# A rational activation's reciprocal moved from ScalarE's logarithm and exponential to VectorE's reciprocal instruction

## The chip, the cores and the metric

One core of one Trainium2 chip runs the whole program. The metric is the device time of one execution in microseconds (us). VectorE is DVE in the profile, ScalarE is ACT, GpSimd is POOL, TensorE is PE.

## The reference

Three stages follow one another over 2 x 4096 = 8192 tokens of width 192: a causal seven-tap convolution along the sequence with softmaxed weights, a layer with a rational activation, and a layer with a squared ReLU. All data is float32.

```
out  = einsum('hk,bskhg->bshg', softmax(weight), windows of x)      # 7 taps
h    = out @ moe_w_in                                               # 192 -> 2048
P    = a[0] + a[1]*h + a[2]*h**2 + a[3]*h**3
Q    = 1.0 + abs(b[0])*abs(h) + abs(b[1])*h**2
g    = P / (Q + 1e-06)
x2   = g @ moe_w_out                                                # 2048 -> 192
y    = (s * relu(x2 @ moe2_w_in)**2 + b2) @ moe2_w_out              # 192 -> 2048 -> 192
```

The change concerns the division in g: 8192 x 2048 reciprocals, which is 128 instructions of 128 partitions x 1024 elements.

## The kernel before

The tokens are cut into 16 tiles of 512 (two batches by eight pieces of the sequence, taken in pairs), and the inner width of 2048 into 8 units of two blocks of 128. So there are 128 units for each layer. A unit n of layer 1 is a tile of 128 x 1024 values of h in PSUM, and every operation on it is one instruction of 128x1024. Everything stays in SBUF and PSUM; only x, the weights and the output are moved by DMA.

Each engine has its own hand-written program (`@block.tensor`, `@block.scalar`, `@block.vector`, `@block.gpsimd`, `@block.sync`), in which a function `phase` goes through the eight units j of a tile; `run` calls it for tiles 0 and 1 written out, for the 12 tiles in the middle in a hardware loop, and for four phases at the end (the last two tiles and two that only empty the pipeline). Semaphores order the engines; inside an engine the order is that of the text. At its step n the work is skewed:

- PE (step n): `first_product` of layer 1 for unit n into `h1` (ten 128x512 matmuls, L314 to L318), the second product of layer 2 for unit n-13 (sixteen matmuls of 192 columns, L340), the first product of layer 2 for unit n-12 (ten, the same lines), the second product of layer 1 for unit n-3 (ten, L327 to L331). `h1` is one buffer: PE waits before `first_product` of unit n until VectorE has finished L615 of unit n-1 (`t3_done`). Layer 2 starts 12 units behind layer 1.
- ScalarE (step n): `a3*h+a2` (L468), `|b1|*|h|` (L470), the rounded high part `gh` of unit n-2 (L477), then for unit n the absolute value of VectorE's product (L480), its logarithm with 1+eps added (L482), the exponential of the negated logarithm, a first estimate of 1/Q (L485), then for layer 2 ReLU (L489) and square (L492).
- VectorE (step n): `(|b1||h| + |b0|) * h` (L610), `t*h` (L612), `(t+a1)*h` (L615), then pieces of the convolution for the next pair of tiles where the table `TAPS_AT` puts them (L510, L513, L521, L524), then for unit n-1 two refining steps, `q = (Q+eps)*r` (L649) and `r = (2-q)*r` (L651), and `g = (P)*r` (L655). At tile bounds it also splits the layer's sums into high and low parts (L570 to L585) and forms the output (L622).
- GpSimd (step n): `gl = g - gh` of unit n-2 (L297).

The buffers `q_buf`, `r_buf` and `num_buf` have two slots each, `gh` and `gl` too. The estimate L485 writes the slot of `r_buf` that `gl` of two units earlier has read, so ScalarE waits on `gl_ready` ahead of it. `w_abs` holds both the result of L470 and the logarithm, so L470 waits on `r0_ready` of the unit before.

Of the kernel before, what the change touches and what calls it, by code (L numbers as in the profile page):

```python
# [8 lines left out]
HALO = TAPS - 1  # L9
EPS_SUM = 1e-9  # L10
EPS_Q = 1e-6
LN_EXP_TABLES = 6

ALU = mybir.AluOpType
ACT = mybir.ActivationFunctionType
# [5 lines left out]
def counted(count):  # L21

    return max(count, 0) if isinstance(count, int) else count


def conv_rational_relu2_kernel(nc, x_main, x_tail, weight, w_in1, w_out1, a, b, w_in2, w_out2, s, b2, out):
# [45 lines left out]
    with ExitStack() as ctx:  # L72
# [6 lines left out]
        def sem(name):  # L79
            return ctx.enter_context(nc.semaphore(name))  # L80
# [19 lines left out]
        w_abs = work1[:, 0]  # L100
        t_buf = work1[:, 7]
        num_buf = [work1[:, 1], work1[:, 2]]
        q_buf = [work1[:, 3], work1[:, 4]]
        r_buf = [work1[:, 5], work1[:, 6]]
# [35 lines left out]
        one_eps = coef[:, 8:9]  # L140
# [23 lines left out]

        h1_ready, t_ready, w_ready = sem("h1_ready"), sem("t_ready"), sem("w_ready")
        z_done, t2_done, t3_done, q_ready = sem("z_done"), sem("t2_done"), sem("t3_done"), sem("q_ready")
        ln_done, r0_ready = sem("ln_done"), sem("r0_ready")
        e_done, r1_done, g_ready = sem("e_done"), sem("r1_done"), sem("g_ready")
        gh_ready, gl_ready, out1_done = sem("gh_ready"), sem("gl_ready"), sem("out1_done")

        h2_ready, u_ready, g2_ready, out2_done = sem("h2_ready"), sem("u_ready"), sem("g2_ready"), sem("out2_done")
# [12 lines left out]
        def raw_tail(c):  # L184

            return raw_w1_tail_early[:, c] if c.stop <= 2 * TOK else raw_w1_tail_late[:, c.start - 2 * TOK:c.stop - 2 * TOK]

        def in_h2(n):

            return isinstance(n, int) and n < SKEW and n % 2 == 1  # L190


        def unit(n):
            return not isinstance(n, int) or 0 <= n < NU

        def tile(t):
            return not isinstance(t, int) or 0 <= t < TILES

        def first(t):
            return isinstance(t, int) and t == 0  # L200

        def second(t):
            return isinstance(t, int) and t == 1
# [5 lines left out]
        def run(eng, phase):  # L209


            for t in range(2):
                phase(t * UNITS, t, t // 2, t % 2)
            with eng.Fori(1, TPB - 1) as i:
                n0 = eng.snap(i * (2 * UNITS))
                t0 = eng.snap(i * 2)
                for parity in range(2):
                    phase(n0 + parity * UNITS, t0 + parity, i, parity)
            for t in range(TILES - 2, TILES + 2):
                phase(t * UNITS, t, t // 2, t % 2)  # L220
# [205 lines left out]
        @block.scalar  # L426
        def _(act):


            act.dma_start(cw[:, :, :], weight).then_inc(cw_loaded, 16)  # L430
            act.add_instruction(mybir.InstLoadActFuncSet(name=nc.get_next_instruction_name(),
                                                         engine=mybir.EngineType.Activation,
                                                         act_func_set_id=LN_EXP_TABLES, ins=[], outs=[]))

            def high_of_weight(dst, raw):
                nc.scalar.copy(dst, raw).then_inc(w_hi_ready, 1)

            def high_of_w1(piece):
                c = PIECES[piece]
                act.wait_ge(w1_loaded[piece], 16)  # L440
                high_of_weight(w1_hi[:, c], raw_w1[:, c])
                act.wait_ge(w1t_loaded[piece], 32)
                high_of_weight(w1_tail_hi[:, c], raw_tail(c))

            act.wait_ge(cw_step, 1)
            nc.scalar.activation(cw[:, :, :], cw[:, :, :], ACT.Exp).then_inc(cw_exp, 1)
            high_of_w1(0)
            act.wait_ge(coef_loaded, 64)
            nc.scalar.activation(coef[:, 4:6], coef[:, 4:6], ACT.Abs).then_inc(coef_ready, 1)
            act.wait_ge(v1_loaded, 16)  # L450
            high_of_weight(v1_hi[:, :, :], raw_v1[:, :, 0:P])
            high_of_weight(v1_tail[:, :, 0, :], raw_v1[:, :, P:D])
            act.wait_ge(coef_ready, 2)

            def phase(n0, t, i, parity):
                for j in range(UNITS):
                    n, m = n0 + j, n0 + (j - SKEW)
                    buf = j % 2
                    if j == X2_STEP and tile(t - 1):

                        act.wait_ge(out1_done, counted(t * UNITS))
                        act.wait_ge(x2_tail_lo_ready, counted(t - 1))
                        nc.scalar.copy(x2_sum, o1_tail[TAIL:P, :]).then_inc(x2_tmp_ready, 1)
                    h_flat = h2_flat if in_h2(n) else h1_flat
                    if unit(n):
                        act.wait_ge(h1_ready, counted(n + 1))
                        act.wait_ge(t3_done, counted(n))
                        nc.scalar.activation(t_buf, h_flat, ACT.Identity, bias=a2, scale=a3).then_inc(t_ready, 1)  # L468
                        act.wait_ge(r0_ready, counted(n))
                        nc.scalar.activation(w_abs, h_flat, ACT.Abs, scale=b1_abs).then_inc(w_ready, 1)  # L470
                    if first(t) and j == 0:
                        high_of_w1(1)
                        high_of_w1(2)
                    if unit(n - 2):
                        act.wait_ge(g_ready, counted(n - 1))
                        act.wait_ge(out1_done, counted(n - 3))
                        nc.scalar.copy(gh[:, buf, :], r_buf[buf]).then_inc(gh_ready, 1)  # L477
                    if unit(n):
                        act.wait_ge(z_done, counted(n + 1))
                        nc.scalar.activation(q_buf[buf], q_buf[buf], ACT.Abs).then_inc(q_ready, 1)  # L480
                        act.wait_ge(q_ready, counted(n + 1))
                        nc.scalar.activation(w_abs, q_buf[buf], ACT.Ln, bias=one_eps).then_inc(ln_done, 1)  # L482
                        act.wait_ge(ln_done, counted(n + 1))
                        act.wait_ge(gl_ready, counted(n - 1))
                        nc.scalar.activation(r_buf[buf], w_abs, ACT.Exp, scale=-1.0).then_inc(r0_ready, 1)  # L485
                    if unit(m):
                        act.wait_ge(h2_ready, counted(m + 1))
                        act.wait_ge(g2_ready, counted(m))
                        nc.scalar.activation(u_relu, h2_flat, ACT.Relu).then_inc(u_ready, 1)  # L489
                        act.wait_ge(u_ready, counted(m + 1))  # L490
                        act.wait_ge(out2_done, counted(m - 1))
                        nc.scalar.activation(g2[buf], u_relu, ACT.Square).then_inc(g2_ready, 1)  # L492
                    if first(t) and j == 4:
                        act.wait_ge(w2_loaded, 16)
                        high_of_weight(w2_hi[:, :], raw_w2)
                    if second(t) and j == 0:
                        act.wait_ge(w2t_loaded, 32)
                        high_of_weight(w2_tail_hi[:, :], raw_w2)

            run(act, phase)  # L500

        @block.vector
        def _(dve):
# [94 lines left out]
            def phase(n0, t, i, parity):  # L598
                for j in range(UNITS):
                    n = n0 + j  # L600
                    buf = j % 2
# [43 lines left out]

                    q, r, num = q_buf[1 - buf], r_buf[1 - buf], num_buf[1 - buf]
                    if unit(n - 1):
                        dve.wait_ge(r0_ready, counted(n))
                        nc.vector.scalar_tensor_tensor(q, q, one_eps, r, ALU.add, ALU.mult).then_inc(e_done, 1)  # L649
                        dve.wait_ge(e_done, counted(n))  # L650
                        nc.vector.scalar_tensor_tensor(r, q, 2.0, r, ALU.subtract, ALU.mult,  # L651
                                                       reverse0=True).then_inc(r1_done, 1)
                        dve.wait_ge(r1_done, counted(n))
                        dve.wait_ge(t3_done, counted(n))
                        nc.vector.scalar_tensor_tensor(r, num, a0, r, ALU.add, ALU.mult).then_inc(g_ready, 1)  # L655
                    if j == X2_STEP and tile(t - 1) and not second(t):
# [2 lines left out]
                    if first(t) and j == 5:  # L659
                        dve.wait_ge(colsum_ready, 1)  # L660
                        nc.vector.tensor_scalar(bias_row[:, :], o2[:, 0, 0, 0:D], b2_col, None,
                                                ALU.mult).then_inc(bias_row_ready, 1)

            run(dve, phase)


# [30 lines left out]
```

## Time and profile before

| | |
|---|---|
| median of 3 executions | 1336.07 us (1335.62 to 1336.43) |
| the profiled execution | 1336.83 us |
| its span, first to last instruction | 1335.0 us |
| PE busy | 1259.8 us (94%) |
| DVE busy | 1160.5 us (87%) |
| ACT busy | 1098.3 us (82%) |
| POOL busy | 333.9 us (25%) |
| mean granted TensorE clock | 0.982 of full speed |

Busy times are sums over one profiled execution. An engine's busy share is an average over the start, the loop and the end; the stretches are told apart in the rows below. Idle time is put down to the instruction that ended it, so a row of waits names who was late.

### The profile page before, as it was taken

To read this page: it belongs to the slowest core of one execution; us is meant where nothing else is said; L and a number is where in the kernel's file an instruction comes from. 1 tells how busy PE (TensorE), PEld (TensorE's weight loads), DVE (VectorE), ACT (ScalarE), POOL (GpSimd) and SP (SyncE) were. 2 spreads that over 40 slices of the span, in tenths; PEclk is the share of its full clock that TensorE was granted. 3 is DMA by queue.
4 is the path that set the end of the run, shared out by engine and by line. 5 is a ranking of instruction groups with operands and counts; after the bars stand their busy time and mean duration, and the time that the engine had idled before them with its cause. 6 is when DMAs were issued, how large, how long until landed. Compare 5 with 4: busy or idle time off the path is not lost.

```text
span 1335.0 us, 16225 instructions
## 1 busy us (share of the span) xinstructions
PE 1259.8 (94%) x5920; PEld 1069.3 (80%) x5920; DVE 1160.5 (87%) x1073; ACT 1098.3 (82%) x1053; POOL 333.9 (25%) x145
## 2 busy tenths in 40 slices
PE   3665899999999999999999999999999999999998
PEld 2544688888888888888888888888888888888887
DVE  7999999998899989999899989999899998978810
ACT  4766788888888888888888888888898888888833
POOL 4233222222222222222222222222222222222200
PEclk9787899999999999999999999999999999999999
DMA  5310100001000100001000010001000000000000
GB/s 134 103 32 0 24 1 12 1 1 36 0 12 0 36 0 0 12 0 36 0 12 0 0 36 0 12 0 36 0 0 12 0 12 1 13 1 13 0 13 12
DMA packets 17885, 20.40 MB, mean 15 GB/s; under 512 B 1472, under 2 KB 13760, under 8 KB 17600
## 3 DMA queue, kind: packets, MB, share of 16 engines
q1 hardware_dynamic: 17712, 20.00, 5.5%
q8 instruction: 18, 0.29, 0.1%
q14 instruction: 11, 0.09, 0.0%
q10 hardware_dynamic: 144, 0.01, 0.0%
HBM read 13.72 MB, written 6.29 MB: 15 GB/s over the span
## 4 chain that ended last, share of the span: by engine, by line
PE 75%; DVE 12%; ACT 6%; issue 5%; POOL 0%; DVEq 0%; ACTq 0%
PE o L340 22%; PE h L314 7%; PE h L317 7%; PE h L315 7%; PE h L316 7%; PE h L318 7%; PE o_tail L329 3%; PE o L327 3%; PE o L328 3%; PE o_tail L331 3%; PE o L330 3%; DVE work L610 3%; DVE work L651 2%; DVE work L649 1%; DVE work L612 1%
## 5 line engine op out<-in xcount | busy, mean ns | idle before, releaser
L297 POOL TENSOR_TENSOR gl<-work,gh 128x1024 fp32r<-128x1024 f32 x128 | 309.1, 2415 | 913.2 <-ACT gh L477 913.2
L340 PE MATMUL o<-v,work 128*128 128x192 f32 x2048 | 355.8, 327 | 3.4 <-ACT work L492 3.4
L340 PEld LDWEIGHTS o<-v,work 128*128 128x128 f32 x2048 | 338.2, 190 | 20.9 <-ACT work L492 11.2
L314 PE MATMUL h<-x_hi,w_hi 128*128 128x512 f32 x512 | 226.5, 442 | 61.5 <-DVE work L615 40.6
L610 DVE SCALAR_TENSOR_TENSOR work<-work,coef,h 128x1024 f32<-128x1024 f32 x128 | 163.6, 1278 | 91.9 <-ACT work L470 91.9
L317 PE MATMUL h<-x_tail,w_tail_hi 128*128 128x512 f32 x512 | 206.6, 403 | 0.0
L315 PE MATMUL h<-x_lo,w_hi 128*128 128x512 f32 x512 | 206.3, 403 | 0.0
L468 ACT ACTIVATE work<-h,coef 128x1024 f32<-128x1024 f32 x128 | 153.9, 1203 | 63.2 <-PE h L318 58.1
L316 PE MATMUL h<-x_hi,w_lo 128*128 128x512 f32 x512 | 205.8, 402 | 0.0
L318 PE MATMUL h<-x_tail,w_tail_lo 128*128 128x512 f32 x512 | 204.6, 400 | 0.0
L480 ACT ACTIVATE work<-work 128x1024 f32<-128x1024 f32 x128 | 135.9, 1062 | 65.7 <-DVE work L610 63.9
L655 DVE SCALAR_TENSOR_TENSOR work<-work,coef 128x1024 f32<-128x1024 f32 x128 | 164.5, 1285 | 4.5
L314 PEld LDWEIGHTS h<-x_hi,w_hi 128*128 128x128 f32 x512 | 98.4, 192 | 87.3 <-issue 38.8
L615 DVE SCALAR_TENSOR_TENSOR work<-work,coef,h 128x1024 f32<-128x1024 f32 x128 | 164.0, 1281 | 4.5
L651 DVE SCALAR_TENSOR_TENSOR work<-work 128x1024 f32<-128x1024 f32 x128 | 161.0, 1258 | 4.4
L649 DVE SCALAR_TENSOR_TENSOR work<-work,coef 128x1024 f32<-128x1024 f32 x128 | 163.9, 1280 | 0.5
L477 ACT CAST gh<-work 128x1024 fp32r<-128x1024 f32 x128 | 134.0, 1047 | 36.7 <-DVE work L655 36.7
L612 DVE TENSOR_TENSOR work<-work,h 128x1024 f32<-128x1024 f32 x128 | 155.3, 1214 | 0.0
L489 ACT ACTIVATE work<-h 128x1024 f32<-128x1024 f32 x128 | 129.1, 1009 | 30.5 <-PE h L318 30.5
L482 ACT ACTIVATE work<-work,coef 128x1024 f32<-128x1024 f32 x128 | 147.7, 1154 | 4.2
L485 ACT ACTIVATE work<-work 128x1024 f32<-128x1024 f32 x128 | 136.0, 1062 | 7.6 <-POOL gl L297 2.9
L470 ACT ACTIVATE work<-h,coef 128x1024 f32<-128x1024 f32 x128 | 141.4, 1104 | 0.0
(62 smaller groups left out, 1563.2 us busy)
## 6 DMA issues: line engine op xcount, KB each, us to landing
out_dram<-y_out SPq DMA_DIRECT2D x16, 384.0 KB, 2.6
xt<-in_x_main_dram SPq DMA_DIRECT2D x7, 518.0 KB, 4.7
xt_tail<-in_x_tail_dram SPq DMA_DIRECT2D x8, 259.0 KB, 5.4
work<-in_moe_w_out_dram SPq DMA_DIRECT2D x1, 1536.0 KB, 10.9
v<-in_moe_w_out_dram SPq DMA_DIRECT2D x1, 1536.0 KB, 7.2
work<-in_moe_w_in_dram SPq DMA_DIRECT2D x1, 1024.0 KB, 9.3
work<-in_moe_w_in_dram SPq DMA_DIRECT2D x2, 512.0 KB, 5.6
xt<-in_x_main_dram SPq DMA_DIRECT2D x2, 259.0 KB, 4.9
```

Of the source, the lines that this page charges most:

```text
L297: nc.gpsimd.tensor_tensor(gl[:, j % 2, :], r_buf[j % 2], gh[:, j % 2, :].bitcast(F32), ALU.subtract).then_inc(gl_ready, 1)
L314: pe.matmul(h[:, half, :], hi[:, c], x_hi[:, :], start=True, stop=False)
L315: pe.matmul(h[:, half, :], hi[:, c], x_lo[:, :], start=False, stop=False)
L316: pe.matmul(h[:, half, :], lo[:, c], x_hi[:, :], start=False, stop=False)
L317: pe.matmul(h[:, half, :], tail_hi[:, c], x_tail[:, :], start=False, stop=False)
L318: last = pe.matmul(h[:, half, :], tail_lo[:, c], x_tail[:, :], start=False, stop=True)
L340: last = pe.matmul(o2[:, c // 2, c % 2, 0:D], g, v2[:, f, :], start=(f == 0 and c % 2 == 0), stop=(f == FT - 1), skip_group_check=True)
L610: nc.vector.scalar_tensor_tensor(q_buf[buf], w_abs, b0_abs, h_flat, ALU.add, ALU.mult).then_inc(z_done, 1)
L612: nc.vector.tensor_tensor(t_buf, t_buf, h_flat, ALU.mult).then_inc(t2_done, 1)
L649: nc.vector.scalar_tensor_tensor(q, q, one_eps, r, ALU.add, ALU.mult).then_inc(e_done, 1)
L651: nc.vector.scalar_tensor_tensor(r, q, 2.0, r, ALU.subtract, ALU.mult, reverse0=True).then_inc(r1_done, 1)
L655: nc.vector.scalar_tensor_tensor(r, num, a0, r, ALU.add, ALU.mult).then_inc(g_ready, 1)
```

## The change

VectorE's reciprocal instruction computes 1/Q. On ScalarE the logarithm (L482) and the exponential (L485) go, and one pass that adds 1+eps to the absolute value comes in; the wait of L470 on the exponential goes. On VectorE the two refining steps (L649, L651) go, and `reciprocal` of 128x1024 comes in ahead of L655; the wait on `gl_ready` moves from ScalarE to VectorE, ahead of the reciprocal. The other engines' programs, the buffers, the convolution's table and the loaded table of functions (number 6) are as before.

```diff
@@ ScalarE, step n
                         nc.scalar.activation(t_buf, h_flat, ACT.Identity, bias=a2, scale=a3).then_inc(t_ready, 1)
-                        act.wait_ge(r0_ready, counted(n))
                         nc.scalar.activation(w_abs, h_flat, ACT.Abs, scale=b1_abs).then_inc(w_ready, 1)
...
                         act.wait_ge(z_done, counted(n + 1))
-                        nc.scalar.activation(q_buf[buf], q_buf[buf], ACT.Abs).then_inc(q_ready, 1)
-                        act.wait_ge(q_ready, counted(n + 1))
-                        nc.scalar.activation(w_abs, q_buf[buf], ACT.Ln, bias=one_eps).then_inc(ln_done, 1)
-                        act.wait_ge(ln_done, counted(n + 1))
-                        act.wait_ge(gl_ready, counted(n - 1))
-                        nc.scalar.activation(r_buf[buf], w_abs, ACT.Exp, scale=-1.0).then_inc(r0_ready, 1)
+                        nc.scalar.activation(q_buf[buf], q_buf[buf], ACT.Abs).then_inc(abs_done, 1)
+                        act.wait_ge(abs_done, counted(n + 1))
+                        nc.scalar.activation(q_buf[buf], q_buf[buf], ACT.Identity, bias=one_eps).then_inc(q_ready, 1)
@@ VectorE, step n, unit n-1
-                        dve.wait_ge(r0_ready, counted(n))
-                        nc.vector.scalar_tensor_tensor(q, q, one_eps, r, ALU.add, ALU.mult).then_inc(e_done, 1)
-                        dve.wait_ge(e_done, counted(n))
-                        nc.vector.scalar_tensor_tensor(r, q, 2.0, r, ALU.subtract, ALU.mult,
-                                                       reverse0=True).then_inc(r1_done, 1)
-                        dve.wait_ge(r1_done, counted(n))
+                        dve.wait_ge(q_ready, counted(n))
+                        dve.wait_ge(gl_ready, counted(n - 2))
+                        nc.vector.reciprocal(r, q).then_inc(r_done, 1)
+                        dve.wait_ge(r_done, counted(n))
                         dve.wait_ge(t3_done, counted(n))
                         nc.vector.scalar_tensor_tensor(r, num, a0, r, ALU.add, ALU.mult).then_inc(g_ready, 1)
```

## Rows read from the trace of the kernel before

**Rows 1.** Stretches: busy us of each engine, instruction count, PEclk, DMA share, GB/s
```profile
core 0: us, PE busy (x) PEld busy (x) DVE busy (x) ACT busy (x) POOL busy (x), PEclk, DMA share, GB/s
0.00:33.00 33.00, 9.80 (x28) 7.10 (x29) 23.87 (x32) 14.32 (x17) 13.04 (x13) 0.98 0.53 136
33.00:167.00 134.00, 90.76 (x335) 71.23 (x334) 128.81 (x113) 96.00 (x90) 42.71 (x18) 0.83 0.15 40
...
300.00:900.00 600.00, 597.84 (x2854) 509.60 (x2854) 550.83 (x510) 524.85 (x503) 149.66 (x63) 1.00 0.04 11
900.00:1200.00 300.00, 298.94 (x1428) 254.74 (x1427) 266.98 (x247) 262.90 (x253) 75.10 (x32) 1.00 0.03 8
```
**Rows 2.** Waits over the span: engine line, releaser, total us, times, longest
```profile
DVE work L610 <- ACT work L470: 91.9, 91, 3.1
...
ACT work L468 <- PE h L318: 58.1, 95, 1.7
```
**Rows 3.** Chain of waits, 683 to 839 us: start us, us, what; two tiles apart
```profile
683.56 2.87 PE o L340 x16
...
838.55 2.87 PE o L340 x16
```
**Rows 4.** DVE timeline, part of one step: start us, us, instruction, idle before
```profile
721.09 1.23 DVE L651 SCALAR_TENSOR_TENSOR work<-work 128x1024 f32<-128x1024 f32 x1
722.36 1.29 DVE L655 SCALAR_TENSOR_TENSOR work<-work,coef 128x1024 f32<-128x1024 f32 x1
724.52 1.28 DVE L610 SCALAR_TENSOR_TENSOR work<-work,coef,h 128x1024 f32<-128x1024 f32 x1 [0.88 <-ACT work L470]
...
730.03 1.28 DVE L649 SCALAR_TENSOR_TENSOR work<-work,coef 128x1024 f32<-128x1024 f32 x1
731.34 1.22 DVE L651 SCALAR_TENSOR_TENSOR work<-work 128x1024 f32<-128x1024 f32 x1
732.60 1.28 DVE L655 SCALAR_TENSOR_TENSOR work<-work,coef 128x1024 f32<-128x1024 f32 x1
```
**Rows 5.** DVE timeline of the weights' softmax at the start
```profile
5.60 0.17 DVE L551 TENSOR_REDUCE cw_sum<-cw 128x2 f32<-128x14 f32 x1 [0.28 <-ACT cw L446]
```
**Rows 6.** DVE groups by line: busy us, mean ns of one, idle before
```profile
L590 DVE TENSOR_TENSOR v_lo<-work,v_hi 128x2048 fp32r<-128x2048 f32 x1 | 2.3, 2292 | 0.0
L548 DVE TENSOR_TENSOR cw<-cw,cw_max 128x14 f32<-128x14 f32 x1 | 0.2, 175 | 0.0
L553 DVE TENSOR_SCALAR cw_sum<-cw_sum 128x2 f32<-128x2 f32 x1 | 0.2, 170 | 0.0
L551 DVE TENSOR_REDUCE cw_sum<-cw 128x2 f32<-128x14 f32 x1 | 0.2, 168 | 0.3 <-ACT cw L446 0.3
L555 DVE RECIPROCAL cw_max<-cw_sum 128x2 f32<-128x2 f32 x1 | 0.2, 166 | 0.0
L583 DVE CAST x_tail<-x_sum 64x512 fp32r<-64x512 f32 x16 | 6.6, 412 | 0.1
```
**Rows 7.** The two stretches on either side of VectorE's last L615 (columns as in rows 1)
```profile
33.00:1259.80 1226.80, 1179.68 (x5532) 999.53 (x5531) 1121.60 (x1027) 1053.47 (x1008) 316.17 (x131) 0.98 0.05 12
1259.80:1335.00 75.20, 70.28 (x364) 62.65 (x362) 15.01 (x16) 30.55 (x30) 4.73 (x2) 1.00 0.04 11
```
**Rows 8.** ACT groups by line: busy us, mean ns of one, idle before
```profile
L468 ACT ACTIVATE work<-h,coef 128x1024 f32<-128x1024 f32 x128 | 153.9, 1203 | 63.2 <-PE h L318 58.1 <-issue 4.7
L482 ACT ACTIVATE work<-work,coef 128x1024 f32<-128x1024 f32 x128 | 147.7, 1154 | 4.2
L470 ACT ACTIVATE work<-h,coef 128x1024 f32<-128x1024 f32 x128 | 141.4, 1104 | 0.0
L485 ACT ACTIVATE work<-work 128x1024 f32<-128x1024 f32 x128 | 136.0, 1062 | 7.6 <-POOL gl L297 2.9
```
**Rows 9.** PE timeline in the first tiles, behind an idle stretch of PE
```profile
103.15 0.63 PE L314 MATMUL h<-x_hi,w_hi 128*128 128x512 f32 x1 [4.37 <-DVE work L615]
103.58 0.63 PE L315 MATMUL h<-x_lo,w_hi 128*128 128x512 f32 x1
...
106.90 0.39 PE L318 MATMUL h<-x_tail,w_tail_lo 128*128 128x512 f32 x1
107.13 0.39 PE L327 MATMUL o<-gh,v_hi 128*128 128x512 f32 x1
```

More of the change, by code:

```diff
@@ L11 @@
 EPS_Q = 1e-6
-LN_EXP_TABLES = 6
+EXP_TABLES = 6
 ALU = mybir.AluOpType
@@ L166, in conv_rational_relu2_kernel @@
         z_done, t2_done, t3_done, q_ready = sem("z_done"), sem("t2_done"), sem("t3_done"), sem("q_ready")
-        ln_done, r0_ready = sem("ln_done"), sem("r0_ready")
-        e_done, r1_done, g_ready = sem("e_done"), sem("r1_done"), sem("g_ready")
+        abs_done, r_done, g_ready = sem("abs_done"), sem("r_done"), sem("g_ready")
         gh_ready, gl_ready, out1_done = sem("gh_ready"), sem("gl_ready"), sem("out1_done")
@@ L432, in _ @@
                                                          engine=mybir.EngineType.Activation,
-                                                         act_func_set_id=LN_EXP_TABLES, ins=[], outs=[]))
+                                                         act_func_set_id=EXP_TABLES, ins=[], outs=[]))
             def high_of_weight(dst, raw):
```

## The prediction

> **What bounds the kernel now.** I read the stretches first. From 300 to 1200 us PE is busy 896.8 of 900 us (597.84 + 298.94) and VectorE 817.8 (550.83 + 266.98), while from 33 to 167 us, where layer 2 has not started or has just done so, VectorE is busy 128.8 of 134 us and PE only 90.8 [rows 1]. So VectorE sets the pace in the first tiles and PE in the loop. The waits say the same: VectorE's largest is L610 on ScalarE's L470, 91.9 us in 91 waits, and ScalarE in its turn waits for PE's first product, 58.1 us [rows 2]. The chain passes the same matmuls 155.0 us later (838.55 - 683.56), which is 16 units, so a unit takes 9.69 us [rows 3]. VectorE works 817.8 / 900 x 9.69 = 8.80 us of it and has **0.89 us of slack per unit**. That slack is what the change has to live with: VectorE may gain work only up to 0.89 us a unit before it becomes the bound.
>
> **What goes.** On VectorE L649 and L651 go. From the start of L649 to the start of L655 they hold the engine for 732.60 - 730.03 = 2.57 us [rows 4]; I take 2.58. On ScalarE the logarithm (1.154 us) and the exponential (1.062 us) go and a pass with a bias comes in; it lies between 1.062 us (a pass from SBUF without bias) and 1.203 us (Identity with scale and bias, from PSUM), and I take L482's 1.154, which has the same operands [rows 8]. ScalarE loses 1.06 us of 787.7 / 900 x 9.69 = 8.48 us per unit [rows 1]. It is not the bound, so this counts as nothing by itself; what covers it is PE now, and VectorE afterwards. The result of the two passes is wanted a step later than it is made, so VectorE does not wait for it. The waits that go with w_abs count as nothing for the same reason, and the moved wait on gl looks at a subtraction two steps back, done long before.
>
> **What comes in.** This is the whole question, because the trace has one RECIPROCAL only, of 128x2: 166 ns [rows 6]. A duration is a fixed part plus elements times a price, so the price is (166 - fixed) / 2, and it hangs on the fixed part:
>
> - TENSOR_SCALAR of the same 128x2 takes 170 ns [rows 6]. By it the elements cost nothing that can be seen; the least I allow is the 1.04 ns below, which makes 1.2 us of an instruction.
> - TENSOR_TENSOR takes 2292 ns for 2048 elements and 175 for 14 [rows 6], so 1.041 ns an element and 160 ns fixed. By it a reciprocal costs 2.8 ns an element, 3.0 us an instruction.
> - TENSOR_REDUCE, which reads one operand of 14 elements and ran two instructions ahead of it [rows 5], takes 168 ns [rows 6], so 168 - 14 x 1.041 = 153 ns fixed. By it: 6.3 ns an element, 153 + 1024 x 6.3 = **6.60 us**.
> - CAST of 64x512 takes 412 ns, which at 1.041 ns an element would leave nothing; it must move two elements in that time, so 412 - 266 = 146 ns is fixed [rows 6]. By it: 10 ns an element, 10.4 us an instruction.
>
> Between 1.2 and 10.4 us I take 6.60. The reduce is the nearest row: like the reciprocal it reads a single SBUF operand at one element a step, writes two elements, and stands in the same idle stretch at the start. 6.3 ns is also six steps of 1.04, an iterating instruction rather than a streaming one.
>
> **The sum**, against the profiled execution's span of 1335.0 us. With 6.60 us VectorE needs 8.80 - 2.58 + 6.63 = 12.85 us a unit (0.03 us stands between L649's end and L651's start, and I give the reciprocal the same), against PE's 9.69. So VectorE becomes the bound everywhere, and its work simply adds up. I cut at 1259.8 us, the end of its last L615. Before the cut it is busy 23.87 + 1121.60 = 1145.5 us [rows 1, 7]. Of that, 126 units' refining steps go, 126 x 2.58 = 325.1, and 126 reciprocals come, 126 x 6.63 = 835.4: 1655.8. The idle time before 33 us, 33 - 23.87 = 9.1 us, is for the loads and the first product and stays. Of the 105 us of idle time between 33 us and the cut [rows 7] I keep 3, for the second tile's splits; the rest was waiting for PE. Behind the cut 75.2 us follow, PE's draining of layer 2. PE no longer arrives with a backlog, which saves about 2. The last two reciprocals lie beside it: the last g comes 6.63 + 1.20 + 6.63 + 1.28 = 15.7 us behind the cut, and with one pass of ScalarE and the subtraction on GpSimd it is at PE some 19 us behind, earlier than PE takes it up now, by some 2 us as I estimate. Sum: 1655.8 + 9.1 + 3 + 73 = 1741 us of span. The profiled execution lies 1.8 us over its span and 0.8 over the median of the runs, so the median becomes **1742 us**, 30% more than before.
>
> **Why VectorE then never waits.** Its order in a step is L610, L612, L615, taps, reciprocal, L655. PE starts unit n+1's first product when L615 of unit n ends, and VectorE needs L470 of unit n+1 next. In between lie at least 6.63 + 1.28 = 7.9 us of its own work. PE needs ten matmuls, then L468 and L470, 2.3 us [rows 8]. Where PE had been idle 4.4 us, the next matmuls came 0.43 us apart, against 0.23 at full speed: its clock was at the lower of its two levels, 1.2 in place of 2.4 GHz, and it was back after 3.7 us of work [rows 9]. So ten matmuls take 2.3 to 4.3 us, and the way is 4.6 to 6.6 us, under 7.9. PE idles some 3.2 us a unit in the new loop, so such half-clock stretches are likely there and the granted clock may drop below 0.9. It costs nothing, as PE's step has room to grow from 9.69 to 12.85 us.
>
> **The rivals.**
>
> - *Eight steps an element.* The same fixed part within the rows' bounds (166 - 2 x 8.33 = 149 ns, between the reduce's 153 and the cast's 146) gives 8.33 ns an element and 8.68 us an instruction. The sum rises by 126 x 2.08 = 262 us: 2004 us. For it: two of four fixed parts enclose it. Against it: the reduce's is nearer in kind. The Trainium skill, VectorE: DVE Perf Modes, section "The DVE is not a fixed-function vector unit" (its "First, the fixed hardware budget"), says that the reciprocal runs as an iterative divide with a repeat count of 8. If that means eight steps for every element, this is its case; no duration is given there, and the row of two elements can't tell six steps from eight.
> - *A middling instruction, 3.0 us.* VectorE would need 8.80 - 2.58 + 3.06 = 9.28 us, inside PE's 9.69; the first 14 units lose 0.5 us each, and steps with two taps overrun: 1340 to 1360 us, or no change at best. Against it: a two-operand instruction's fixed part.
> - *A streaming instruction, 1.2 us: faster.* Place and price: only the first 14 units, where VectorE is the bound, gain 1.35 us each, 19 us; the loop is PE's and gives back at most its 3.2 us of idle in 900, and the end 2. That is 1312 us. It decides below 2.58 us an instruction, so below 2.4 ns an element. For it: the TENSOR_SCALAR of the same shape took longer than the reciprocal did (170 against 166 ns). Against it: that row would leave a negative price for two elements.
> - *A dearer instruction, 10.4 us* by the cast: 1742 + 126 x 3.8 = 2221 us, and beyond.
>
> **How the numbers follow.** Chances: forecast 0.47, eight steps 0.32, middling 0.06, streaming 0.08, dearer 0.07. The range holds the first two with some room on both sides: 1660 us is a reciprocal of 5.95 us, 2040 one of 8.97. That leaves out about 0.2. A measurement of this kernel can tell about 0.2% from no change; faster by more is the streaming case, 0.08, within it a third of the middling one, 0.02, slower the rest, 0.90.
>
> **What would show it.** In the new profile the group of 128 RECIPROCALs of 128x1024 has a mean near 6600 ns and is by far VectorE's largest, 845 us; 8700 or 1200 decide for a rival at once. VectorE is busy 95% or more, with no waits worth naming at L610; PE is at 72 to 76%, its largest wait being L314 on VectorE's L615; ScalarE is near 960 us. The clock's mean falls below 0.98. The prediction is wrong in its mechanism if VectorE is under 93% busy, which would mean a new wait on PE's slower clock or on ScalarE, and wrong only in a size if the time is VectorE's old work plus 126 times another duration.

## The result, and the profile after

| | before | after |
|---|---|---|
| median | 1336.25 us (1335.62 to 1338.1, 4 runs) | 1745.23 us (1744.96 to 1745.82, 4 runs) |
| ratio | | 1.3058, interval 1.3036 to 1.3081 |
| span of the profiled execution | 1335.0 us | 1743.1 us |
| mean granted TensorE clock | 0.982 | 0.906 |

The kernel became 409 us slower, where 406 had been forecast. The first part of the new page shows whose work grew:

```profile
PE 1391.6 (80%) x5920; PEld 1146.4 (66%) x5920; DVE 1666.7 (96%) x945; ACT 977.3 (56%) x925; POOL 329.1 (19%) x145
```

VectorE went from 87% to 96% with 128 instructions fewer. PE has the same 5920 matmuls and more busy time, 1391.6 against 1259.8 us, which is the lower clock. Among VectorE's groups (line, operation, shape and count, then busy us, mean ns of one, idle time before them) the new one is first by a factor of five; L648, L605 and L610 are the L655, L610 and L615 of before:

```profile
L645 DVE RECIPROCAL work<-work 128x1024 f32<-128x1024 f32 x128 | 838.1, 6548 | 0.5
L648 DVE SCALAR_TENSOR_TENSOR work<-work,coef 128x1024 f32<-128x1024 f32 x128 | 164.5, 1285 | 4.5
L610 DVE SCALAR_TENSOR_TENSOR work<-work,coef,h 128x1024 f32<-128x1024 f32 x128 | 164.0, 1281 | 4.5
L605 DVE SCALAR_TENSOR_TENSOR work<-work,coef,h 128x1024 f32<-128x1024 f32 x128 | 163.1, 1275 | 3.0 <-ACT work L468 2.4
...
L550 DVE RECIPROCAL cw_max<-cw_sum 128x2 f32<-128x2 f32 x1 | 0.2, 166 | 0.0
```

One reciprocal of 128x1024 takes 6548 ns. The neighbours kept their durations, so it disturbs nobody; they only stand in its queue. The small instance of [rows 6] takes 166 ns here as before (L550, the L555 of before). The idle time before L605 (L610 of before), 91.9 us in [rows 2], is down to 3.0. In the stretches (columns as in [rows 1]) VectorE is full from 33 us on:

```profile
33.00:167.00 134.00, 70.80 (x224) 54.32 (x224) 133.00 (x73) 57.85 (x53) 31.89 (x14) 0.75 0.11 34
300.00:900.00 600.00, 494.78 (x2129) 407.23 (x2128) 595.54 (x336) 348.21 (x330) 112.24 (x47) 0.92 0.03 7
900.00:1500.00 600.00, 499.89 (x2124) 412.10 (x2124) 595.48 (x335) 349.80 (x331) 109.82 (x46) 0.91 0.02 7
```

The waits (who waited for whom, total us, times, longest) turned round. PE and ScalarE now wait for VectorE, PE at layer 1's first product (L313) and ScalarE at the high part of g (L475). The last row is what is left of the old order, ScalarE waiting for PE:

```profile
ACT gh L475 <- DVE work L648: 444.7, 125, 10.0
PEld h L313 <- DVE work L610: 235.5, 96, 7.2
PE h L313 <- DVE work L610: 222.5, 89, 9.9
ACT work L467 <- PE h L317: 178.6, 115, 3.3
```

A step in VectorE's timeline (start us, us, instruction), with nothing between the instructions; one that waits for nothing even starts 0.08 or 0.09 us before the one in front has ended (922.70 + 1.28 = 923.98 against 923.90):

```profile
922.70 1.28 DVE L648 SCALAR_TENSOR_TENSOR work<-work,coef 128x1024 f32<-128x1024 f32 x1
923.90 1.28 DVE L605 SCALAR_TENSOR_TENSOR work<-work,coef,h 128x1024 f32<-128x1024 f32 x1
925.09 1.22 DVE L607 TENSOR_TENSOR work<-work,h 128x1024 f32<-128x1024 f32 x1
926.34 1.28 DVE L610 SCALAR_TENSOR_TENSOR work<-work,coef,h 128x1024 f32<-128x1024 f32 x1
927.54 1.28 DVE L508 SCALAR_TENSOR_TENSOR conv<-xt,cw,conv 128x1024 f32<-128x1024 f32 x1
928.73 6.55 DVE L645 RECIPROCAL work<-work 128x1024 f32<-128x1024 f32 x1
```

One view misleads here. The chain that ended last gives

```profile
issue 56%; DVE 24%; POOL 15%; PE 3%; ACT 1%; DMA 0%; POOLq 0%; DVEq 0%; ACTq 0%
```

as if GpSimd and bare issuing set the time. Its pieces in the loop alternate between GpSimd's subtraction and long stretches of "issue": it follows the reciprocal's second wait, on `gl_ready`, which guards the slot of `r_buf`. The timeline says that this wait was met long before. The subtraction that began at 910.84 us took 2.39 us, so it ended at 913.23, and that slot is written again only by the second reciprocal behind it, at 928.73. The one between began at 916.12. Both stand right behind VectorE's own instructions. VectorE is busy 595.5 of 600 us (99%), so it waits for nobody, and that decides over the chain.

### The profile page after: what moved, and what is told of

The parts are those of the page before. It is cut to its first block, busy times and chain, and to the rows that moved or that the text cites. A ratio compares the mean times of both kernels' runs of the same rounds, so it can differ in the third digit from the quotient of the medians.

```text
span 1743.1 us, 15969 instructions
## 1 busy us (share of the span) xinstructions
PE 1391.6 (80%) x5920; PEld 1146.4 (66%) x5920; DVE 1666.7 (96%) x945; ACT 977.3 (56%) x925; POOL 329.1 (19%) x145
## 4 chain that ended last, share of the span: by engine, by line
issue 56%; DVE 24%; POOL 15%; PE 3%; ACT 1%; DMA 0%; POOLq 0%; DVEq 0%; ACTq 0%
DVE work L645 16%; POOL gl L296 15%; DVE work L648 2%; PE o L339 2%; DVE work L605 2%; DVE work L607 1%; ACT gh L475 1%; DVE conv L508 1%; DVE conv_tail L519 0%; PE h L313 0%; PE h L316 0%; PE h L315 0%; PE h L314 0%; PE h L317 0%; DMA cw<-in_weight_dram 0%
## 5 line engine op out<-in xcount | busy, mean ns | idle before, releaser
L645 DVE RECIPROCAL work<-work 128x1024 f32<-128x1024 f32 x128 | 838.1, 6548 | 0.5
L313 PE MATMUL h<-x_hi,w_hi 128*128 128x512 f32 x512 | 256.5, 501 | 295.6 <-DVE work L610 222.5
L475 ACT CAST gh<-work 128x1024 fp32r<-128x1024 f32 x128 | 134.6, 1051 | 445.0 <-DVE work L648 444.7
L339 PEld LDWEIGHTS o<-v,work 128*128 128x128 f32 x2048 | 352.9, 196 | 13.6
L313 PEld LDWEIGHTS h<-x_hi,w_hi 128*128 128x128 f32 x512 | 108.5, 212 | 359.9 <-DVE work L610 235.5
L314 PE MATMUL h<-x_lo,w_hi 128*128 128x512 f32 x512 | 227.0, 443 | 0.0
L315 PE MATMUL h<-x_hi,w_lo 128*128 128x512 f32 x512 | 224.8, 439 | 0.0
L316 PE MATMUL h<-x_tail,w_tail_hi 128*128 128x512 f32 x512 | 223.9, 437 | 0.0
L317 PE MATMUL h<-x_tail,w_tail_lo 128*128 128x512 f32 x512 | 221.7, 433 | 0.0
L648 DVE SCALAR_TENSOR_TENSOR work<-work,coef 128x1024 f32<-128x1024 f32 x128 | 164.5, 1285 | 4.5
L610 DVE SCALAR_TENSOR_TENSOR work<-work,coef,h 128x1024 f32<-128x1024 f32 x128 | 164.0, 1281 | 4.5
L605 DVE SCALAR_TENSOR_TENSOR work<-work,coef,h 128x1024 f32<-128x1024 f32 x128 | 163.1, 1275 | 3.0 <-ACT work L468 2.4
L484 ACT ACTIVATE work<-h 128x1024 f32<-128x1024 f32 x128 | 129.3, 1010 | 39.6 <-PE h L317 39.5
L326 PE MATMUL o<-gh,v_hi 128*128 128x512 f32 x256 | 107.9, 422 | 51.7 <-DVE x_lo L567 40.5
```

The costliest lines, as they stand in the source:

```text
L313: pe.matmul(h[:, half, :], hi[:, c], x_hi[:, :], start=True, stop=False)
L314: pe.matmul(h[:, half, :], hi[:, c], x_lo[:, :], start=False, stop=False)
L315: pe.matmul(h[:, half, :], lo[:, c], x_hi[:, :], start=False, stop=False)
L316: pe.matmul(h[:, half, :], tail_hi[:, c], x_tail[:, :], start=False, stop=False)
L317: last = pe.matmul(h[:, half, :], tail_lo[:, c], x_tail[:, :], start=False, stop=True)
L339: last = pe.matmul(o2[:, c // 2, c % 2, 0:D], g, v2[:, f, :], start=(f == 0 and c % 2 == 0), stop=(f == FT - 1), skip_group_check=True)
```

## The experiments

Each edit is against the changed kernel unless it says the kernel before. Times are medians; where a ratio stands, it is to the kernel before on the same chip. `...` stands for lines left out.

**What one reciprocal costs.** Behind the last instruction of the kernel before stand, each waiting for the one in front:

```diff
+            nc.vector.memset(t_buf, 3.0).then_inc(cw_step, 1)
+            dve.wait_ge(cw_step, 2)
+            nc.vector.reciprocal(w_abs[:, 0:64], t_buf[:, 0:64]).then_inc(cw_step, 1)
+            dve.wait_ge(cw_step, 3)
...
+            nc.vector.reciprocal(w_abs[:, 0:1024], t_buf[:, 0:1024]).then_inc(cw_step, 1)
+            dve.wait_ge(cw_step, 7)
+            nc.vector.tensor_tensor(w_abs[:, 0:64], t_buf[:, 0:64], t_buf[:, 0:64], ALU.mult).then_inc(cw_step, 1)
+            dve.wait_ge(cw_step, 8)
+            nc.vector.tensor_tensor(w_abs[:, 0:1024], t_buf[:, 0:1024], t_buf[:, 0:1024], ALU.mult).then_inc(cw_step, 1)
```

> The kernel before with five reciprocals of 64, 128, 256, 512 and 1024 elements of the value 3.0 and two products of 64 and 1024 elements behind its last instruction on VectorE, each waiting for the one in front. Theory A (six steps of 1.04 ns an element, 0.15 us fixed, whatever the value): 0.55, 0.95, 1.75, 3.35 and 6.55 us. Rival 1 (a price that grows with size, by a fixed part of 0.17 us and batches): the points leave a line by over 2%. Rival 2 (the price depends on the data, and 3.0 is a cheap or a dear value): the 1024 elements take other than 6.55 us. The products give 1.04 ns an element and 0.16 us.

VectorE's timeline behind the end of the kernel:

```profile
1332.08 0.55 DVE L667 RECIPROCAL work<-work 128x64 f32<-128x64 f32 x1
1332.66 0.95 DVE L669 RECIPROCAL work<-work 128x128 f32<-128x128 f32 x1
1333.65 1.75 DVE L671 RECIPROCAL work<-work 128x256 f32<-128x256 f32 x1
1335.44 3.35 DVE L673 RECIPROCAL work<-work 128x512 f32<-128x512 f32 x1
1338.83 6.55 DVE L675 RECIPROCAL work<-work 128x1024 f32<-128x1024 f32 x1
1345.41 0.22 DVE L677 TENSOR_TENSOR work<-work 128x64 f32<-128x64 f32 x1
1345.67 1.23 DVE L679 TENSOR_TENSOR work<-work 128x1024 f32<-128x1024 f32 x1
```

All five lie on one line: (6.55 - 0.55) / 960 = 6.25 ns an element and 0.55 - 64 x 6.25 / 1000 = 0.15 us fixed. The products give (1.23 - 0.22) / 960 = 1.05 ns. So an element costs six times what it costs in a product. The constant 3.0 takes as long as the kernel's varied data. The 2-element row of before was on the same line: between it and the kernel's 1024 elements lie (6548 - 166) / 1022 = 6.24 ns an element, which leaves 153 ns fixed.

**The same elements in two instructions.**

```diff
-                        nc.vector.reciprocal(r, q).then_inc(r_done, 1)
+                        nc.vector.reciprocal(r[:, 0:TOK], q[:, 0:TOK])
+                        nc.vector.reciprocal(r[:, TOK:W], q[:, TOK:W]).then_inc(r_done, 1)
```

> The changed kernel with each reciprocal cut into two of 128x512. Theory A (VectorE's work adds up, price per element 6.25 ns and a fixed part of about 0.15 us): each half takes about 3.35 us, a unit gains 0.07 to 0.18 us (the two may overlap a little), 126 units gain 9 to 23 us: 1754 to 1768 us. Theory B (part of the time is a wait of VectorE on PE at its lower clock or on ScalarE): the extra work is swallowed by that wait, 1745 to 1750 us.

Measured: 1746.47 us (1745.92 to 1747.5), ratio 1.307 (1.3048 to 1.3091). That is 1 us more, and so no difference that this measurement tells. Theory A's range was missed, but Theory B did not win by it; the timeline shows why:

```profile
903.81 3.35 DVE L645 RECIPROCAL work<-work 128x512 f32<-128x512 f32 x1
907.08 3.30 DVE L646 RECIPROCAL work<-work 128x512 f32<-128x512 f32 x1
910.41 1.28 DVE L649 SCALAR_TENSOR_TENSOR work<-work,coef 128x1024 f32<-128x1024 f32 x1
```

From the first to L649 it is 6.60 us, against 6.57 for the single instruction (908.39 - 901.82). Without a wait between them the second starts before the first has ended, and most of the fixed part is hidden. There was hardly any extra work in this kernel (0.03 us in each of 126 steps, 4 us), so it does not tell the theories apart; the next ones do.

**One streaming pass in the reciprocal's place.** It leaves out the division.

```diff
-                        nc.vector.reciprocal(r, q).then_inc(r_done, 1)
+                        nc.vector.tensor_tensor(r, q, q, ALU.mult).then_inc(r_done, 1)
```

> The changed kernel with one streaming pass (q*q, 128x1024) in place of the reciprocal; it leaves out the division. Theory A: the pass takes 1.2 us, VectorE needs 7.45 us of work per unit and PE is the bound again at 9.6 us; only the start gains: 1312 us, the time of the streaming rival. Theory B: the changed order of waits costs by itself, so the time stays above 1340 us although VectorE has less to do than before.

Measured: 1310.25 us (1308.9 to 1312.68), ratio 0.9808 (0.9792 to 0.9824). The pass takes 1237 ns, PE is busy every microsecond from 300 to 900 us, and VectorE's wait for ScalarE is back at 231.1 us, larger than before the change:

```profile
300.00:900.00 600.00, 600.00 (x2880) 515.42 (x2880) 478.27 (x453) 464.61 (x448) 152.74 (x63) 1.00 0.03 9
...
DVE work L605 <- ACT work L468: 231.1, 111, 3.4
```

So everything else in the change, the removed and moved waits and ScalarE's lighter step, does no harm that this run shows. The whole loss is the instruction's duration. The streaming rival's 1312 us was met to 2 us, though by terms that cancel: by unit 16 the kernel is 15.3 us ahead of the kernel before, not 19, and another 10 come in the loop, not 3.

**A reciprocal inside PE's slack.** It leaves out the division for 576 of 1024 columns. The reciprocal works in place, so VectorE also waits for its own g ahead of the next step's first instruction (L605, here L606).

```diff
+                        dve.wait_ge(g_ready, counted(n - 1))
...
-                        nc.vector.reciprocal(r, q).then_inc(r_done, 1)
+                        nc.vector.reciprocal(q[:, 0:448], q[:, 0:448]).then_inc(r_done, 1)
...
-                        nc.vector.scalar_tensor_tensor(r, num, a0, r, ALU.add, ALU.mult).then_inc(g_ready, 1)
+                        nc.vector.scalar_tensor_tensor(r, num, a0, q, ALU.add, ALU.mult).then_inc(g_ready, 1)
```

> The changed kernel with the reciprocal on 448 of the 1024 columns only, and one more wait of VectorE on its own g; it leaves out the division for the other columns. Theory A: the instruction takes 2.95 us, a unit of VectorE's work about 9.3 us, which is inside PE's 9.69: 1340 to 1360 us, with PE near 98% busy in the loop. A line straight through the changed kernel's time would give 1745 - 126 x 3.6 + 10 = 1301 us, which a bound by PE excludes. Theory B (slow clock of PE matters as soon as VectorE is close to the bound): above 1380 us.

Measured: 1349.62 us (1348.52 to 1349.95), ratio 1.0098 (1.0081 to 1.0115); the instruction took 2946 ns. As Theory A had it, PE is nearly full again and VectorE close behind:

```profile
300.00:900.00 600.00, 591.98 (x2824) 503.95 (x2824) 572.49 (x444) 457.69 (x437) 147.78 (x61) 1.00 0.04 11
```

This is the middling rival's case, at a time within its range: 576 columns less bring the time back to PE's, but not quite to the 1336 us of before. By the mean, 8.80 - 2.58 + 2.98 = 9.2 us a step, VectorE would never hold PE up; but L606 waits for ScalarE in only 52 of its 128 steps:

```profile
DVE work L606 <- ACT work L468: 48.3, 52, 3.2
```

In the other 76 VectorE has no time to spare. There the added wait costs too: L606 begins 0.13 us behind the end of g (725.13 against 723.71 + 1.28) and not 0.08 ahead of it. That is 0.2 us a step and up to 76 x 0.2 = 15 us, about as much as the 13 us by which this kernel is slower than the one before. So this run does not say what the 448 columns alone would cost.

**More work for ScalarE.**

```diff
+        extra_done = sem("extra_done")
...
                         act.wait_ge(g2_ready, counted(m))
+                        if unit(n):
+                            nc.scalar.activation(u_relu, h2_flat, ACT.Relu).then_inc(extra_done, 1)
+                            act.wait_ge(extra_done, counted(m * 2 + 1))
+                            nc.scalar.activation(u_relu, h2_flat, ACT.Relu).then_inc(extra_done, 1)
+                            act.wait_ge(extra_done, counted(m * 2 + 2))
```

> The changed kernel with two more passes of ScalarE (ReLU of 128x1024, about 2.2 us) in each of 116 steps. Theory A (ScalarE's relief was worth nothing): ScalarE rises to about 9.6 us of VectorE's 12.8, the time stays within 3 us of 1745. Rival (ScalarE's passes lie on the way to L605): up to 116 x 2.2 = 255 us more, 1850 to 2000 us.

Measured: 1746.68 us (1745.81 to 1747.15), ratio 1.3073 (1.3051 to 1.3095). ScalarE is busy 437.84 in place of 348.21 us of the same 600 and the time does not move by more than the measurement tells. With the reciprocal in place ScalarE's relief of 1.06 us is worth nothing, as the sum had it.

**More and less work for PE.** More: layer 2's first product is computed twice.

```diff
-                last.then_inc(done, 1)
+                if done is not None:
+                    last.then_inc(done, 1)
...
+                        if unit(n):
+                            first_product(h2, k2, w2_hi, w2_lo, w2_tail_hi, w2_tail_lo,
+                                          x2_hi[x2p], x2_lo[x2p], x2_tail[x2p], None)
                         first_product(h2, k2, w2_hi, w2_lo, w2_tail_hi, w2_tail_lo,
```

> The changed kernel with layer 2's first product computed twice in 116 steps, ten more matmuls. Theory A (PE's step has room to grow from 9.6 to 12.8 us): the loop takes PE 12.0 us at full clock, still inside; 1745 to 1760 us, PE over 92% busy in the loop and the granted clock nearer 1.0 as PE idles less. Theory B (PE's slow stretches are on the path): well over 1780 us, at most 1745 + 116 x 2.3 = 2012 us.

Less: both first products lose a matmul, which leaves out the correction by `w_lo`.

```diff
-                    pe.matmul(h[:, half, :], lo[:, c], x_hi[:, :], start=False, stop=False)
```

> The changed kernel without one of the five matmuls of the two first products (w_lo with x_hi), 4 fewer per step; it leaves out that correction term. Theory A: no change in the loop; only the drain of layer 2 behind VectorE's last unit is shorter, 12 units by 0.46 us: about 1739 us. Theory B (the way over PE at its lower clock counts): 2 matmuls fewer on the way to L605 at 0.23 to 0.43 us each, 60 to 110 us less.

Measured: 1764.32 us with more (ratio 1.3205, 1.3183 to 1.3227) and 1740.07 us with less (1.3022, 1.3 to 1.3044). Their stretches from 300 to 900 us, the one with more first:

```profile
300.00:900.00 600.00, 563.88 (x2594) 472.52 (x2593) 589.10 (x330) 349.96 (x330) 110.99 (x46) 0.98 0.03 8
```

```profile
300.00:900.00 600.00, 470.14 (x1936) 389.45 (x1935) 595.54 (x336) 347.66 (x330) 111.82 (x47) 0.88 0.03 7
```

With less, VectorE is busy the same 595.54 us and only the drain is shorter: 5.2 us less in all, where 5.5 had been reckoned. The granted clock fell further, to 0.88 here, and that cost nothing. With more, PE is 94% busy and the clock is up at 0.98, as expected, but the time lies 4 us over the range of Theory A. The loss is there when VectorE ends its last L614 (the L610 of the changed kernel), at 1685.5 in place of 1666.8 us; what follows takes as long as without the added matmuls. VectorE now has waits, for ScalarE's second pass over h, which in its turn waits for PE:

```profile
DVE work L609 <- ACT work L472: 19.7, 22, 2.9
```

Most of them stand at tile bounds. There layer 2 begins a new tile, and its first product needs the `x_tail` that VectorE has just split (L584):

```profile
1544.34 0.69 DVE L584 TENSOR_TENSOR x_tail<-x_sum,x_tail 64x512 fp32r<-64x512 f32 x1
1545.34 0.47 PE L313 MATMUL h<-x_hi,w_hi 128*128 128x512 f32 x1 [3.90 <-issue]
...
1558.79 1.28 DVE L609 SCALAR_TENSOR_TENSOR work<-work,coef,h 128x1024 f32<-128x1024 f32 x1 [1.17 <-ACT work L472]
...
1570.69 1.28 DVE L609 SCALAR_TENSOR_TENSOR work<-work,coef,h 128x1024 f32<-128x1024 f32 x1 [0.39 <-ACT work L472]
```

PE stands 3.9 us, has its 12 us of work still before it, and the h of the next unit comes late. In the changed kernel the same wait (3.9 us at 911.04) did no harm. By the starts of L609 and of L605 in the two traces, 14 such bounds make 14.8 of the 18.8 us. Another 3.4 come in the last tiles, where seven steps without convolution take PE's 11.91 us (1570.69 - 1558.79 = 11.90) for VectorE's 11.43 (1651.62 - 1640.19, between two L605 near the changed kernel's end). Over all steps VectorE's mean is higher than PE's work, but a step that PE can't finish in time is not made good by the mean.

**The same cut in the kernel before.**

> The same cut in the kernel before. Theory A (PE is the bound in its loop, VectorE 0.89 us behind): a unit falls from 9.69 us by 0.92 us to about VectorE's 8.80: 1225 to 1250 us. Rival (the loop before is bound by the round of waits PE to ScalarE to VectorE and not by PE's work): 2 matmuls less in the round, 0.46 us a unit, about 1280 us.

Measured: 1289.96 us (1289.5 to 1290.93), ratio 0.9656 (0.964 to 0.9672). Both figures were missed, the rival's 1280 by less. PE's share falls to 572.74 of 600 us, so its work was the bound and no longer is; VectorE's is 569.02. VectorE's timeline shows steps of 9.28 us (from 702.75 to 712.03, here L609 is the L610 of before) where two pieces of the convolution stand in them, with no wait inside:

```profile
702.75 1.28 DVE L609 SCALAR_TENSOR_TENSOR work<-work,coef,h 128x1024 f32<-128x1024 f32 x1 [0.34 <-ACT work L469]
...
712.03 1.27 DVE L609 SCALAR_TENSOR_TENSOR work<-work,coef,h 128x1024 f32<-128x1024 f32 x1
```

The mean of 8.80 us hid that. It is not the whole account, since in 65 of its steps VectorE still waits for ScalarE:

```profile
DVE work L609 <- ACT work L469: 52.9, 65, 2.3
```

Theory C of the last run takes up VectorE's long steps alone.

**Both cuts.** The kernel before without its refining steps, and then without the correction by `w_lo` too.

```diff
-                        nc.vector.scalar_tensor_tensor(q, q, one_eps, r, ALU.add, ALU.mult).then_inc(e_done, 1)
-                        dve.wait_ge(e_done, counted(n))
-                        nc.vector.scalar_tensor_tensor(r, q, 2.0, r, ALU.subtract, ALU.mult,
-                                                       reverse0=True).then_inc(r1_done, 1)
-                        dve.wait_ge(r1_done, counted(n))
```

> The kernel before without its two refining steps; it leaves out the refining of the estimate of 1/Q. Theory A: PE is the bound in the loop, so 2.58 us less per unit on VectorE gains only in the first 14 units, 30 to 35 us, and some 3 us in the loop: about 1300 us. Rival (VectorE's steps lie on the way from the first product to the next in the loop too): 1336 - 128 x 0.3 or more, below 1290 us.

> The kernel before without its two refining steps and without the matmul of w_lo with x_hi in the two first products; it leaves out the refining and that correction term. Theory C (in the cut kernel before, VectorE's steps with convolution taps, 9.3 us long, took over as the bound in those steps, which is why it gained 46 and not 105 us): with 2.58 us off every VectorE step the whole 0.92 us per unit appears, 1303.7 - 114 x 0.92 = 1199 us, up to 1220 as ScalarE at 8.5 us a unit comes close behind PE's 8.8. Rival (the round of waits PE, ScalarE, VectorE set the cut kernel's pace, not VectorE's work): about 1303.7 - 46 = 1258 us.

Measured: 1303.71 us without refining (1303.55 to 1304.02, ratio 0.9757, 0.9741 to 0.9773), and 1236.84 us with both (1236.4 to 1237.2, ratio 0.9255, 0.9239 to 0.927). The first is Theory A's: PE is busy 600.00 of 600 us, so 2.58 us less per step on VectorE, 330 us of its work, gave 32.5 us. Of these 22.9 are there by the L610 of unit 16, in the kernel before and without refining:

```profile
182.16 1.28 DVE L610 SCALAR_TENSOR_TENSOR work<-work,coef,h 128x1024 f32<-128x1024 f32 x1 [2.07 <-ACT work L470]
```

```profile
159.25 1.28 DVE L610 SCALAR_TENSOR_TENSOR work<-work,coef,h 128x1024 f32<-128x1024 f32 x1 [4.66 <-ACT work L470]
```

The other 10 come in the loop, where 3 had been expected: a unit takes 9.59 us there in place of 9.68 (from unit 16 to 120 in the two traces). PE's 3.2 us of idle time in 900 did not show all that it had to give; where the rest lay no run tells.

The second lies between the theories' figures. Relieving VectorE did free part of what the cut alone had not given (66.9 us against 46.3), but PE is not the bound again:

```profile
300.00:900.00 600.00, 589.75 (x2786) 490.89 (x2785) 424.99 (x416) 557.96 (x538) 159.96 (x67) 1.00 0.04 11
```

ScalarE's timeline there shows it as the next one. It goes through its eight passes without a gap worth naming but one, the 0.48 us in which L479 waits for VectorE's product, and comes round every 9.0 us (715.50 - 706.58 = 8.92, 724.56 - 715.50 = 9.06):

```profile
706.58 1.21 ACT L467 ACTIVATE work<-h,coef 128x1024 f32<-128x1024 f32 x1
...
710.20 1.06 ACT L479 ACTIVATE work<-work 128x1024 f32<-128x1024 f32 x1 [0.48 <-DVE work L609]
...
715.50 1.20 ACT L467 ACTIVATE work<-h,coef 128x1024 f32<-128x1024 f32 x1
...
724.56 1.20 ACT L467 ACTIVATE work<-h,coef 128x1024 f32<-128x1024 f32 x1
```

So of the 0.92 us that PE gained per step, ScalarE's round lets 0.6 through. That is read from the timeline: PE is busy 98% of this stretch and ScalarE 93%, and no run took work off ScalarE here. Theory C's 1199 to 1220 us was missed by 17. Both kernels are faster than the two of the study, at the price of what they leave out.

## Why the prediction was right

The mechanism and the price held, and the sum came out within 3 us. The sum by its own terms, with the same cut behind VectorE's last L610 (L615 of before), where these stretches of the changed kernel lie:

```profile
0.00:33.00 33.00, 9.37 (x27) 6.97 (x28) 24.38 (x32) 14.88 (x17) 12.96 (x13) 0.95 0.53 136
33.00:1666.70 1633.70, 1311.18 (x5536) 1076.52 (x5535) 1621.41 (x902) 933.08 (x881) 311.40 (x131) 0.90 0.03 9
1666.70:1743.00 76.30, 71.05 (x358) 62.92 (x358) 20.92 (x14) 29.35 (x29) 4.79 (x2) 0.98 0.04 11
```

| term | forecast, us | measured, us |
|---|---|---|
| VectorE busy ahead of the cut | 1655.8 | 24.38 + 1621.41 = 1645.8 |
| idle before 33 us | 9.1 | 33 - 24.38 = 8.6 |
| idle from 33 us to the cut | 3 | 1633.70 - 1621.41 = 12.3 |
| behind the cut | 73 | 76.4 |
| span | 1741 | 1743.1 |

- **The price of the reciprocal** was the step on which all hung: 6.60 us forecast, 6.548 measured. It came from one row of 166 ns and the choice of the reduce's fixed part, 153 ns, and that choice was exact. It was also lucky in part: with the cast's 146 ns, 7 ns less, the same row gave 10.4 us. A price from two elements multiplies an error of one nanosecond by 512. What was safe in the forecast was its sign, which four of the five prices shared, one of them barely; its size hung on this one choice, to which the prediction gave 0.47.
- **VectorE's own sum** was 10 us too high, by three errors. Busy time counts an overlap once, and the prediction took times from start to start, with the gap, for busy time. A reciprocal adds 6.548 - 0.08 = 6.47 us and not 6.63, which makes 126 x 0.16 = 20 us less. A refining pair had 2.45 us of its own and not 2.58, so 126 x 0.13 = 16 us too much was taken off. And L605, which had followed a wait 91 times, now overlaps L648 by 0.08 us, 7 us less.
- **Idle time to the cut** was too low, 3 for 12.3 us. There are no large waits in it. It is 4.5 us in every 600, the gaps of some 0.03 us in front of an instruction that waits for VectorE's own last result (4.5 us in all ahead of L610, 4.5 ahead of L648). The trace of before has them too, within its 105 us, and I had thrown them away with the waits for PE.
- **The drain** did not get shorter by 2 us but longer by 1.2. PE arrives without a backlog, but it then stood 2.3 us, 0.9 of them behind the cut, for ScalarE's ReLU (L484), and came back at the lower clock, with its matmuls 0.43 us apart:

```profile
1667.56 0.50 PE L313 MATMUL h<-x_hi,w_hi 128*128 128x512 f32 x1 [2.32 <-ACT work L484]
...
1668.63 0.63 PE L316 MATMUL h<-x_tail,w_tail_hi 128*128 128x512 f32 x1
1669.06 0.63 PE L317 MATMUL h<-x_tail,w_tail_lo 128*128 128x512 f32 x1
```

  In ScalarE's order that ReLU stands behind the two passes on VectorE's late product, so the late VectorE reached PE by way of ScalarE's queue. I had looked at the last g only. VectorE had it done at 1682.3 us, 15.6 behind the cut as forecast, but PE took it up at 1689.3, 22.6 behind the cut, where the kernel before took it up 21.4 behind (1281.2 - 1259.8).

These three misses have both signs and nearly cancel; the 3 us between forecast and median is luck, and better than the terms deserve.

- **The clock.** After 3.9 us of idle time PE's matmuls come 0.43 us apart again (911.61, 912.03), the half-clock spacing of [rows 9]. The loop's clock fell to 0.91. Cutting PE's work took it to 0.88, more work for ScalarE or PE raised it, to 0.97 and 0.98, and VectorE's 595.54 busy us in 600 stayed the same at 0.88, 0.92 and 0.97. That the clock costs nothing is shown for the loop. It does not hold in the drain, where PE is what the time hangs on: from 1668.20 to 1671.19 seven spacings took 3.0 us, at 0.23 each they would have taken 1.6. The forecast of 72 to 76% for PE's busy share was 1259.8 us of work at the old clock; at the lower one the same matmuls were busy 1391.6 us, 80%. Why more work for ScalarE raised the clock no run shows.
- **VectorE never waits** held: 3.0 us of idle time ahead of all 128 L605.
- **The rivals.** The middling and the streaming case were built and came out at 1350 and 1310 us, against 1340 to 1360 and 1312. The eight steps an element are out: it is six. The repeat count of 8 that the Trainium skill gives for the reciprocal (VectorE: DVE Perf Modes, "First, the fixed hardware budget") can't be read as time per element here; the five sizes give 6.25 ns, six of VectorE's 1.04 ns steps. What the count stands for no run here shows.
- **The slack of 0.89 us** was right as a mean and wrong as a bound for each step. In the kernel with 448 columns and in the cut kernel before, VectorE waits in some steps (52 and 65 waits) and sets the pace in others. With ten more matmuls for PE the same is true from the other side: steps at tile bounds wait for PE although VectorE's mean step is the longer one.

## What to carry to other kernels

Before an operation is replaced by a "single instruction", get its price per element, not its count: the reciprocal of 1024 float32 elements costs five of the passes that it was to save two of. If the trace has one small instance, set its duration beside a neighbour with the same kind of operands to find the fixed part, and carry the error of that choice through to the time. An engine's slack under another's bound is a matter of each step, not of the mean, and once the engine has none left in any step, each microsecond that a step gains counts in full. A busy share adds overlaps once, so take the price of an instruction in a full queue from start to start.

## What the runs showed of the hardware

- VectorE's reciprocal on float32 costs 6.25 ns an element from 64 to 1024 elements, with 0.15 us fixed, for a constant as for the kernel's data.
- Two reciprocals of 512 elements with no wait between them took 6.60 us where one of 1024 took 6.57: the second's fixed part is hidden behind the first.
- ScalarE's passes kept their time beside a VectorE that is at its reciprocal half of the time: its ReLU of 128x1024 (L484) took 1010 ns on average, against 1009 before.
- After 3.9 us of idle time PE's matmuls of 512 columns came 0.43 us apart, and 0.23 later in the same burst (from 917.13 us on).
